# The x^T of batches 2 to 4 by scratch memory and VectorE block transposes instead of TensorE transposes, with two edits of the first batch

## What is computed

```
state = alpha[t][:, None] * state + outer(k[t], v[t]);  x[t] = q[t] @ state        # attention, per head
h = relu(x.T @ w_tok1) @ w_tok2;   u = x + h.T                                      # token mixer (768 -> 256 -> 768)
x2 = u + relu(u @ w_ch1) @ w_ch2                                                    # channel mixer (384 -> 1536 -> 384)
out = sigmoid(xr @ w_r) * (relu(xk @ w_k) ** 2 @ w_v)                               # xk, xr: mu * x2 + (1 - mu) * x2 one token before
```

## Time and profile before

| | |
|---|---|
| median of 3 runs | 739.76 us |
| the profiled execution | 739.7 us |
| its span, first to last instruction | 737.9 us |
| first batch alone | about 0 to 57 us of the span |
| mixers of batch 1, 2, 3 beside attention of 2, 3, 4 | about 57 to 414 us |
| mixers of batch 4 | about 414 to 498 us |
| last layer | 498 us to the end |

### The profile page before, as it was taken

How to read it: one execution, slowest core, us unless ns; L and a number is a source line. 1 busy time by engine, 2 the same in 40 slices (tenths; PEclk the granted TensorE clock), 3 DMA queues, 4 the chain that set the end, 5 groups by cost and what they waited for, 6 DMA issues and landing times.

```text
span 737.9 us, 13805 instructions
## 1 busy us (share of the span) xinstructions
PE 731.2 (99%) x4598; PEld 724.0 (98%) x4598; DVE 460.4 (62%) x1279; ACT 330.9 (45%) x943; POOL 197.5 (27%) x344
## 2 busy tenths in 40 slices
PE   8999999999999999999999999999999999999998
PEld 7899999999999999999999999999999999999998
DVE  6987878764877873887874321446356374473561
ACT  4866544432544442544443232335455374363551
POOL 3874555341224443223434340320000000000000
PEclk9999999999999999999999999999999999999999
DMA  9974443421424331243430024010011010110000
GB/s 201 209 138 100 86 55 73 55 36 41 58 37 57 70 52 22 58 58 40 79 70 1 33 86 139 33 33 34 33 44 53 32 33 32 53 43 32 11 21 32
DMA packets 174042, 43.82 MB, mean 59 GB/s; under 512 B 161312, under 2 KB 171168, under 8 KB 173984
## 3 DMA queue, kind: packets, MB, share of 16 engines
q1 hardware_dynamic: 170736, 37.98, 25.8%
q0 software_dynamic: 1152, 4.72, 1.7%
q10 hardware_dynamic: 2096, 0.39, 0.3%
HBM read 33.63 MB, written 9.44 MB: 58 GB/s over the span
## 4 chain that ended last, share of the span: by engine, by line
PE 95%; DVE 2%; ACT 2%; DMA 1%; issue 0%; SPq 0%; DVEq 0%
PE bank L745 21%; PE bank L761 20%; PE bank L838 14%; PE bank L816 14%; PE bank L825 5%; PE bank L662 4%; PE bank L733 3%; PE bank L630 3%; PE bank L701 3%; PE bank L667 2%; PE bank L660 2%; PE bank L724 1%; PE bank L625 1%; PE bank L638 1%; PE bank L713 1%; ACT x_half L919 1%
## 5 line engine op out<-in xcount | busy, mean ns | idle before, releaser
L925 ACT ACTIVATE hid_hi<-bank 128x384 fp32r<-128x384 f32 x96 | 47.2, 492 | 118.2 <-PE bank L745 118.2
L1182 DVE SCALAR_TENSOR_TENSOR hid_lo<-bank,hid_hi 128x384 fp32r<-128x384 f32 x96 | 53.3, 555 | 68.0 <-ACT hid_hi L925 66.9
L1027 ACT ACTIVATE relu_k<-bank 128x384 f32<-128x384 f32 x64 | 31.6, 493 | 105.9 <-PE bank L816 86.0
L745 PE MATMUL bank<-u_hi,wch_hi 128*128 128x384 f32 x288 | 72.2, 359 | 0.0
L745 PE MATMUL bank<-u_lo,wch_hi 128*128 128x384 f32 x288 | 66.3, 338 | 0.0
L761 PE MATMUL bank<-hid_lo,wch_hi 128*128 128x384 f32 x288 | 65.5, 334 | 0.0
L745 PE MATMUL bank<-u_hi,wch_lo 128*128 128x384 f32 x288 | 65.5, 334 | 0.0
L761 PE MATMUL bank<-hid_hi,wch_hi 128*128 128x384 f32 x288 | 65.4, 334 | 0.0
L761 PE MATMUL bank<-hid_hi,wch_lo 128*128 128x384 f32 x288 | 65.4, 334 | 0.0
L516 POOL TENSOR_SCALAR_AFFINE_SELECT relu_k<-relu_k 128x256 f32<-128x256 f32 x72 | 29.4, 409 | 120.3 <-ACT relu_k L907 120.2
L1292 DVE TENSOR_TENSOR x_half<-bank,x_half 128x384 f32<-128x384 f32 x24 | 13.4, 557 | 77.3 <-PE bank L838 75.3
(11 more groups left out here) (135 smaller groups left out, 1837.3 us busy)
## 6 DMA issues: line engine op xcount, KB each, us to landing
w_raw<-in_moe_w_ch SPq DMA_DIRECT2D x12, 384.0 KB, 3.6
x_scratch<-x_half POOLq DMA_DIRECT2D x8, 576.0 KB, 3.5
out<-x_half SPq DMA_DIRECT2D x24, 192.0 KB, 1.9
vt<-in_v SPq DMA_DIRECT2D x48, 72.0 KB, 2.2
qka<-in_q SPq DMA_DIRECT2D x49, 48.0 KB, 2.2
qka<-in_alpha SPq DMA_DIRECT2D x49, 48.0 KB, 2.2
qka<-x_scratch SPq DMA_DIRECT2D x4, 577.5 KB, 3.9
qka<-in_k SPq DMA_DIRECT2D x48, 48.0 KB, 2.2
```

Of the source, the lines that this page charges most:

```text
L745: mm = nc.tensor.matmul(dst, ch1_w(a, n % KC, jj), u[c][:, n % KC, half * HT:(half + 1) * HT], start=(n == 0), stop=(n == 3 * KC - 1))
L925: nc.scalar.activation(dst, b_ring[t % 2][:, 0:HT], func).then_inc(tile_hi, 1)
L1182: ins = nc.vector.scalar_tensor_tensor(dst, src, 0.0, hi, ALU.max, ALU.subtract)
```

## The change

x^T of batches 2 to 4 (index 1 to 3) is no longer made by TensorE. Each chunk of `x_sum` is stored to the scratch memory of x2, loaded again in four DMAs which exchange the 32x32 blocks, and one DVE instruction for each chunk then transposes within the blocks (`turn_x`, into `x2_half[0]` or the first half of `x_sum`). DVE adds the result while it empties a token-down bank (`down_base`), which writes u itself into `x2_half`; ACT makes u hi from that and POOL u lo. Batch 1 keeps the TensorE transposes, with a copy in place of the addition. Further: q, k and alpha of step 1 of batches 3 and 4 are prepared one slot earlier; POOL's list of slots for the w_ch2 half-pieces is moved; in the first batch the order of the first loads, the counts of dummy products and the splitting of weights (in halves, one in each slot) change.

```diff
+    TURN_SLOT = SLOTS - 4
+    LOW_SLOT = 10
+        x_rows = [x2_dram[b].rearrange("d s -> (d s)").rearrange("(t c) -> t c", c=DM) for b in range(B)]
+        xT = [x2_half[0][:, :, :], x_sum[:, 0:KC, :]]
         def prepared(r, s):
-            if s == SLOTS - 2:
-                return (r + 1, 0) if r + 1 < B else None
+            if s >= SLOTS - 2:
+                return (r + 1, s - SLOTS + 2) if r + 1 < B else None
             i = step_in(s, 0)
-            return None if i is None else (r, i)
+            return None if i is None or (i == 1 and r > 1) else (r, i)
...
+            def arrange_x(b, c):
+                n = NC * (b - 1) + c + 1
+                rows = x_rows[b][c * P:(c + 1) * P, :]
+                sp.wait_ge(x_sum_ready, n)
+                sp.dma_start(rows, x_sum[:, c, :]).then_inc(x_rows_stored, 16)
+                sp.wait_ge(x_rows_stored, 16 * n)
+                for a in range(4):
+                    sp.dma_start(x_sum[32 * a:32 * (a + 1), c, :].rearrange("p (m t j) -> p m t j", m=KC, j=32),
+                                 rows.rearrange("(t p) (m a j) -> a p m t j", p=32, a=4, j=32)[a])\
+                      .then_inc(x_raw_loaded[c], 16)
...
-            for n, t in ((0, q), (2, alpha)):
-                sp.dma_start(qka3[0][n][:, 2:H, 0:D], t[0, 2:H, 0:P, :].rearrange("h p d -> p h d"))\
-                  .then_inc(qka_loaded[0], 16)
-            for c in range(3):
-                if c > 0:
-                    load_qka(c)
-                    load_v(c)
-                for n in range(2 * c, min(2 * c + 2, NRAW)):
-                    load_piece(n)
+            sp.dma_start(qka3[0][0][:, 2:H, 0:D], q[0, 2:H, 0:P, :].rearrange("h p d -> p h d"))\
+              .then_inc(qka_loaded[0], 16)
+            load_v(0)
+            for c in range(1, 3):
+                load_qka(c)
+                load_piece(c - 1)
+                load_v(c)
+            load_piece(2)
...
                     load_half(r, n)
                     if r == 1 and n == 2:
                         load_piece(NMIX - 2)
+                    if r > 1 and n < 2:
+                        arrange_x(r - 1, 3 * n)
+                        if n == 1:
+                            arrange_x(r - 1, 4)
                     load_half_v(r, n)
+                    if r > 1 and n == 0:
+                        arrange_x(r - 1, 1)
+                        arrange_x(r - 1, 2)
+                    if r > 1 and n == 1:
+                        arrange_x(r - 1, 5)
                     if r == 1 and n == 2:
                         load_piece(NMIX - 1)
+            for c in range(NC):
+                arrange_x(B - 1, c)
...
-            HALF_SLOT = (1, 1, 3, *range(5, NJ + 2))
+            HALF_SLOT = (3, *range(5, NJ + 4))
-            def prepare_x2(b, n):
+            def down_low(b, n):
...
+                pool.wait_ge(tile_hi, TILES * b + KT + n + 1)
+                nc.gpsimd.tensor_tensor(u[1][:, m, us], x2_half[half][:, m, :], u[0][:, m, us], ALU.subtract)\
+                    .then_inc(u_lo_ready, 1)
...
-                if BASE_SLOT <= s < BASE_SLOT + 2 * KC:
-                    prepare_x2(r - 1, s - BASE_SLOT)
+                for n in range(2 * KC):
+                    if s == (1 + n // 2 if n < KC else LOW_SLOT + n - KC):
+                        down_low(r - 1, n)
...
-            WARM = (4, 2, 1, 1, 1, 1, 1)
+            WARM = (4, 4, 2, 3, 2, 1, 1)
...
-                if m == 0 and b > 0:
-                    pe.wait_ge(x_sum_ready, NC * (b - 1) + TM * (half + 1))
-                for n in range(TM):
-                    nc.tensor.matmul(dst[:, n * P:(n + 1) * P], x_sum[:, TM * half + n, m * P:(m + 1) * P], ident[:, :],
-                                     start=(n == 0), stop=False, is_transpose=True)
+                if b == 0:
+                    for n in range(TM):
+                        nc.tensor.matmul(dst[:, n * P:(n + 1) * P], x_sum[:, TM * half + n, m * P:(m + 1) * P],
+                                         ident[:, :], start=(n == 0), stop=False, is_transpose=True)
...
                 if jj == 0:
-                    pe.wait_ge(tile_lo, TILES * b + KT + KC * (half + 1) + 2)
+                    pe.wait_ge(u_lo_ready, 2 * KC * b + KC * (half + 1))
...
-                tile_second(r - 1, s)
                 if r == 1 and s > 0 and s % 2 == 0 and s < NJ:
                     split_hi(CH1_END + s // 2)
                 if prep is not None:
                     spread_q(*prep)
+                tile_second(r - 1, s)
...
-                tile_high(b, KT + n, u[0][:, m, half * HT:(half + 1) * HT], ACT.Copy)
+                act.wait_ge(tile_lo, TILES * b + KT + n + 3)
+                nc.scalar.activation(u[0][:, m, half * HT:(half + 1) * HT], x2_half[half][:, m, :], ACT.Copy)\
+                    .then_inc(tile_hi, 1)
...
-            act.dma_start(qka3[0][1][:, 2:H, 0:D], k[0, 2:H, 0:P, :].rearrange("h p d -> p h d"))\
-               .then_inc(qka_loaded[0], 16)
-            act.dma_start(vt3[0].rearrange("p (h d) -> p h d", h=H),
-                          v[0, :, 0:P, :].rearrange("h p d -> p h d")).then_inc(v_loaded[0], 16)
+            for n, t in ((1, k), (2, alpha)):
+                act.dma_start(qka3[0][n][:, 2:H, 0:D], t[0, 2:H, 0:P, :].rearrange("h p d -> p h d"))\
+                   .then_inc(qka_loaded[0], 16)
             for s in range(SLOTS):
                 head_part(s)
-                for n in pieces_in(s):
-                    split_hi(n)
+                n, half = divmod(s - 3, 2)
+                if 0 <= n < CH1_END:
+                    split_half_hi(n, half)
...
+                turn_x_part(r, s)
+            def turn_x_part(r, s):
+                if s >= TURN_SLOT and r < B:
+                    turn_x(r, s - TURN_SLOT)
+                if s < 2 and r > 1:
+                    turn_x(r - 1, SLOTS - TURN_SLOT + s)
...
+            def turn_x(b, c):
+                n = NC * (b - 1)
+                dve.wait_ge(x_raw_loaded[c], 64 * b)
+                if c == 0:
+                    dve.wait_ge(x2_stored[0], 16 * b)
+                if c == TM:
+                    dve.wait_ge(x_turned, n + TM)
+                half, k = divmod(c, TM)
+                nc.vector.transpose(xT[half][:, :, k * P:(k + 1) * P],
+                                    x_sum[:, c, :].rearrange("p (m f) -> p m f", m=KC)).then_inc(x_turned, 1)
+            def down_base(b, n):
+                half, m = divmod(n, KC)
+                t = KT + n
+                src = b_ring[t % 2][:, 0:HT]
+                dve.wait_ge(tile_done, TILES * b + t + 1)
+                if b == 0:
+                    ins = nc.vector.tensor_copy(x2_half[half][:, m, :], src)
+                else:
+                    if m == 0:
+                        dve.wait_ge(x_turned, NC * (b - 1) + TM * (half + 1))
+                        dve.wait_ge(x2_stored[half], 16 * b)
+                    ins = nc.vector.tensor_tensor(x2_half[half][:, m, :], src, xT[half][:, m, :], ALU.add)
+                ins.then_inc(tile_lo, 1)
```

More of the change, by code:

```diff
@@ L207, in attention_mixer_channel_mix @@
         acc_read = sem("acc_read")
-        x2_base = sem("x2_base")
+        u_lo_ready = sem("u_lo_ready")
+        x_rows_stored = sem("x_rows_stored")
+        x_raw_loaded = [sem(f"x_raw_loaded{n}") for n in range(NC)]
+        x_turned = sem("x_turned")
         x2_stored = [sem(f"x2_stored{n}") for n in range(2)]
@@ L376, in load_piece @@
                 if n >= NALL - NLATE:
-                    sp.wait_ge(tile_done, TILES * (B - 1) + KT + 2 * KC)
+                    sp.wait_ge(tile_lo, TILES * (B - 1) + KT + 2 * KC + 2)
                 elif n >= NRAW:
@@ L507, in add_x @@
                 if c == 0:
-                    pool.wait_ge(tile_done, TILES * (r - 1) + KT + 2 * KC)
+                    pool.wait_ge(tile_lo, TILES * (r - 1) + KT + 2 * KC + 2)
                 pool.wait_ge(xlo_ready, STEPS * (r + 1) - NC + c + 1)
@@ L575, in _ @@
             for n in range(2 * KC):
-                prepare_x2(B - 1, n)
+                down_low(B - 1, n)
             for n in range(NMIX, WR_END):
@@ L733, in token_down @@
                     mm = nc.tensor.matmul(dst, h1[i][:, kt, m * P:(m + 1) * P], tok2_w(j, kt, half),
-                                          start=False, stop=(n == 3 * KT - 1))
+                                          start=(b > 0 and n == 0), stop=(n == 3 * KT - 1))
                 mm.then_inc(tile_done, 1)
@@ L866, in split_hi, with split_half_hi @@
                 nc.scalar.activation(dst[0][:, off:off + rows * cols], raw, ACT.Copy).then_inc(w_hi_ready, 1)
+            def split_half_hi(n, half):
+                _, dst, off = PIECES[n]
+                raw, loaded, value = staging(n)
+                act.wait_ge(loaded, value)
+                cols = slice(half * DM, (half + 1) * DM)
+                ins = nc.scalar.activation(dst[0][:, off + half * DM:off + (half + 1) * DM], raw[:, cols], ACT.Copy)
+                if half == 1:
```

(23 more changed lines are left out.)

4 lines of the change are left out of this document (removed).

## The result

The changed kernel takes 764.88 us (median of 5 runs, 764.04 to 766.8) beside 739.76 for the kernel before on the same chip: a ratio of 1.0348, 95% interval 1.0336 to 1.036, so 25 us slower, where 6 us had been foretold. The profiled execution has a span of 763.2 us.

What follows compares the result with a forecast made beforehand. PE (TensorE) was taken as the bound, so removed PE work shortens the time and PE waits lengthen it; -5.6 + 5.2 + 1.6 + 6.0 - 1.2 = +6.0 on 739.8 gave 745.8 us, range 738.5 to 751.5.

Steps and rivals of the forecast that it cites:

- first batch: Start of batch 1: earlier alpha, added dummy products and weights split in halves save 1.2 us, range -3.0 to +0.5.
- transposes of 18 tiles: Token-down tiles of three batches: removing the three PE transposes in each saves 5.6 us, one tile gaining nothing.
- batch 2, moved splits: SP, held at w_ch2 piece gates, loads late for steps 6 and 9; PE waits add 1.6 and 5.2 us.
- two passages: Into batches 3 and 4: chunk round trips on SP make chunk 5 late before slot 3, +3.0 us each, +6.0 together.
- rival 3: After batch 2's long wait PE runs at half rate: 747.9 us, up to 752 if passages do too; chance 0.22.
- Batch 4's mixers: Only chunks are on SP there, each with two slots for its round trip; all come in time, costing nothing.
- only delays h low and the x2 store, and PE needs neither yet: Passages, end of slot 27: DVE waits 5 us for chunk 3, at no cost to PE.

## Why the prediction failed, step by step

The runs give each term of the sum by itself, in time:

| term | foretold | measured | from |
|---|---|---|---|
| first batch | -1.2 | -1.7 | 739.63 to 737.93 |
| transposes of 18 tiles | -5.6 | -5.85 | 737.93 to 732.08 |
| batch 2, moved splits | +5.2 + 1.6 = +6.8 | +7.5 | 732.08 to 739.61 |
| two passages | +6.0 | +25.3 | 739.61 to 764.88 |

The runs come from different chips, on which the kernel before took 739.33 to 739.76 us, so a row is good to some 0.4 us. The second row is all that the change brings beyond the first batch once its waits are gone.

The first three hold. The mechanism of batch 2 is as written: piece 15 released by the split in slot 9, `load_half(1, 3)` behind it, 4.01 us of waiting where 4.0 to 6.2 were given, and 1.33 three slots before where 0.95 to 3.0 were given. That the term comes so near is in part luck: the waits are 5.3 us where 6.8 were taken, and the half rate behind step 7 adds 1.6 (the outputs of steps 7 and 8 start 6.06 us apart, 4.42 in the kernel before), which the sum had left to rival 3 at a price of 2.1. Batch 4's mixers lose nothing, as foretold.

**The step that failed is "+3.0 for each of the two passages".** Its mechanism was right, SP's row of round trips with chunk 5 at the end, and the term was mis-sized four to one. Shifted by the 6.0 us that batch 2 had lost by then, chunk 5 was to land at 183.1 + 6.0 = 189.1; it was there at 196.1. The 7.0 us are these:
- A chunk costs SP 4.95 us and not 4.05: four chunks ahead, 3.6 us. Its four loads hold SP 2.6 us (0.625 us each, median of 72), where I took 2.1 from loads of another pattern; a store lands in 2.3 us (median of 18, up to 4.6), where I took the 1.9 of another line.
- `load_half(2, 1)` took 7.4 us and not 6.2, as one group of issues stretched to 3.14: 1.2 us.
- Chunk 5 itself needed 196.1 - 188.5 = 7.6 us and not 5.7, and v 0.2 more: 2.1 us.

With a wait of 2.4 + 7.0 = 9.4 us in place of 2.4, and the slow products behind it, some 3 us, a passage comes to 12.4; the trace has 10.1 + 2.0 = 12.1 in the first and 13.2 in the second (the 2.0 are the transposes that each passage saves). So a chain of five round trips multiplied an error of 0.9 us each. The doubt that I had added, one or two stretched issues and a high end of 4.5, was that of single events, and left no room for every link being dearer.

**A second sentence failed: that a late chunk 3 "only delays h low and the x2 store, and PE needs neither yet".** It was 8.34 us late and not 5, and PE did stop for h low, 2.08 + 0.70 us. That this adds nothing to the time, as chunk 5 comes later anyway, follows from SP's rows and is not shown by a run.

**Rival 3, the slow clock, was a rival and should have been a term.** It stood at 747.9 us with the long wait of batch 2 alone and at up to 752 with the passages; the trace has it in both passages: of 25.3 us there, 14.3 are waits (5.9 and 8.4) and the other 11 slow products, some 5 of these ahead of chunk 5's landing (3.1 and 1.9) and so inside a time that SP sets. Even its 752 is 13 us short, so the clock is not the step that failed first. The Trainium skill, "TensorE: Matmul & The Clock Gate", section "HAM oscillation — how this bites in real kernels", says that a PE left idle starts its next burst cold. The trace agrees: the granted clock is 0.72 and 0.79 in the windows of the passages, and 1.00 from 206 to 312 us between them.

## What to carry to other kernels

A term that stands on a queue's serial work is a sum over its whole row: price each kind of issue and each landing by its own pattern, and multiply the doubt by the number of links, since here the errors all had one sign. When one queue both stores, waits for the landing and loads, move the store to the queue of the engine that made the data: here that, and changes in the order of SP's loads, turned a loss of 25 us into a gain of 7.3. Where PE is the bound, a wait of a few us is to be priced with the slow products that may stand behind it: 1.6 us behind the 4.01 of step 7.

## What was not expected of the hardware

The issue time of a DMA did not follow its size: on SP a load of 48 KB in pieces of 128 bytes into 32 partitions holds the queue 0.625 us (median of 72), one of 48 or 24 KB of q, k or alpha 0.47, the store of a chunk of 192 KB 0.61, a load of 384 KB of w_ch 0.45 (median of 12). Single ones were stretched, in the changed kernel up to 1.28 us (chunk loads), 1.73 (q, k, alpha), 1.82 (chunk stores) and 0.91 (w_ch). POOL's store of the same chunk took 0.56 to 0.61 us of its queue and landed in 2.4 to 2.6 (medians of three runs; from SP 2.3). PE lost its clock behind single idle stretches of 2.42, 2.46, 3.13, 3.83, 4.01 and 5.79 us, and behind 1.86 or 2.08 followed by 0.70; it kept it behind 1.10, 1.33, 1.57, 1.77 and, at the token-up of the runs with POOL's stores, 2.00 and 2.11. One case does not fit that order: in the run with dummies in the passages the clock fell behind 1.39 us at step 4 of batch 2 (products 0.32 us apart from 83.95 on, granted clock 0.50 from 84 to 86). So between 1.39 and 2.11 us the length of a wait alone did not tell whether slow products would follow.
